# The first sixteen steps of an attention and two-MLP kernel on two tiles of TensorE, with four smaller edits

## The reference, cut to what matters

```
q, k, v: batch 4, heads 8, seq 576, head_dim 64
scores = (q @ k^T) / 8
thresh = max(scores, -1) - tau
scores = where(scores >= thresh, scores, -1e9) - max(scores)
attn   = exp(scores) / (sum(exp(scores)) + 1e-9)
x      = attn @ v                       -> x: 2304 tokens x 512
h  = x @ w_in;   g  = h * sigmoid(1.702 h);      x2  = g @ w_out    (d_ff 2048)
h2 = x2 @ w_in2; g2 = h2 * tanh(softplus(h2));   out = g2 @ w_out2
```

## Time and profile before

| | |
|---|---|
| median of 3 runs | 1164.04 us (1163.72 to 1164.51) |
| the profiled execution's own time | 1164.05 us |
| its span, first to last instruction | 1162.3 us |
| busy PE / PEld / DVE / ACT / POOL | 96 / 89 / 65 / 62 / 25 % |
| mean granted clock of TensorE | 0.995 |
| PE in the slices, tenths | 8978889999999999999999999999999999999998 |

### The profile page before, as it was taken

The page is one execution under the profiler, slowest core; times in us unless marked ns, Lnnn a source line. Parts: engine busy times, 40 slices in busy tenths (PEclk is TensorE's granted clock), DMA queues, the critical chain, the costliest instruction groups (busy, mean ns, idle before and its releaser), DMA issues.

```text
span 1162.3 us, 19359 instructions
## 1 busy us (share of the span) xinstructions
PE 1118.1 (96%) x7472; PEld 1035.4 (89%) x7472; DVE 759.1 (65%) x1359; ACT 724.1 (62%) x995; POOL 295.4 (25%) x502
## 2 busy tenths in 40 slices
PE   8978889999999999999999999999999999999998
PEld 4568889998999999999999999998999989899997
DVE  4678788888888888888888434665433444344343
ACT  3678787767777777777767322467545554554453
POOL 3557674434444433344333000000000000000000
PEclk9989999999999999999999999999999999999999
DMA  2443534232143222233231003520010000000000
GB/s 65 140 131 114 158 86 111 59 94 85 48 111 91 64 82 77 79 105 83 70 103 28 26 19 106 190 76 28 6 49 1 28 28 28 28 28 28 1 28 27
DMA packets 92923, 78.71 MB, mean 68 GB/s; under 512 B 47520, under 2 KB 78752, under 8 KB 92832
## 3 DMA queue, kind: packets, MB, share of 16 engines
q1 hardware_dynamic: 92832, 77.49, 22.9%
HBM read 63.83 MB, written 13.63 MB: 67 GB/s over the span
## 4 chain that ended last, share of the span: by engine, by line
PE 78%; DVE 11%; ACT 7%; issue 3%; POOL 0%; DMA 0%; SPq 0%; ACTq 0%; DVEq 0%
PE ps_s L743 17%; PE ps_r L628 14%; PE ps_r L648 11%; PE ps_r L766 9%; PE ps_t L492 6%; PE ps_t L513 5%; PE ps_t L766 4%; PE ps_s L477 4%; PE ps_t L648 3%; PE ps_r L513 2%; PE ps_s L466 2%; DVE x_pair L585 2%; DVE pt_lo L574 2%; ACT pv_half_sb L544 1%; DVE neg_max L554 1%
## 5 line engine op out<-in xcount | busy, mean ns | idle before, releaser
L628 PE MATMUL ps_r<-x_hi,wi_lo 128*128 128x256 f32 x544 | 158.5, 291 | 2.7 <-DVE x_lo L701 2.7
L810 DVE COPY hidden<-ps_s 128x768 f32<-128x768 f32 x48 | 45.8, 956 | 170.5 <-PE ps_s L743 170.5
L628 PE MATMUL ps_r<-x_lo,wi_hi 128*128 128x256 f32 x544 | 154.2, 284 | 0.0
L628 PE MATMUL ps_r<-x_hi,wi_hi 128*128 128x256 f32 x544 | 154.2, 283 | 0.0
L492 PE MATMUL ps_t<-ident,e_buf 128*128 128x128 f32 x720 | 118.1, 283 | 27.1 <-DVE pt_lo L574 14.5
L839 ACT ACTIVATE m_lo_raw<-m_lo_raw 128x1536 f32<-128x1536 f32 x24 | 35.8, 1491 | 168.8 <-DVE m_lo_raw L817 168.8
L561 DVE SCALAR_TENSOR_TENSOR e_buf<-ps_s,neg_thr,e_buf 128x576 f32<-128x576 f32 x144 | 117.0, 813 | 29.4 <-ACT e_buf L521 22.9
L648 PE MATMUL ps_r<-g_hi,wo_lo 128*128 128x256 f32 x464 | 135.4, 292 | 0.0
L537 ACT CAST pt_hi<-ps_t 128x640 fp32r<-128x640 f32 x128 | 89.0, 695 | 71.8 <-PE ps_t L492 69.6
L743 PE MATMUL ps_s<-x_hi,wi_lo 128*128 128x384 f32 x384 | 129.0, 336 | 2.4 <-DVE x_lo L799 2.4
L492 PEld LDWEIGHTS ps_t<-ident,e_buf 128*128 128x128 f32 x720 | 84.7, 143 | 52.1 <-issue 29.2
(11 more groups left out here) (105 smaller groups left out, 3009.9 us busy)
## 6 DMA issues: line engine op xcount, KB each, us to landing
k_ll_raw<-in_k SPq DMA_DIRECT2D x56, 288.0 KB, 2.9
v_st_raw<-in_v SPq DMA_DIRECT2D x64, 160.0 KB, 2.9
wi_lo_raw<-in_moe_w_in SPq DMA_DIRECT2D x16, 512.0 KB, 3.8
wo_lo_raw<-in_moe_w_out SPq DMA_DIRECT2D x16, 512.0 KB, 4.8
q_raw<-in_q SPq DMA_DIRECT2D x32, 192.0 KB, 2.9
x_scratch<-y_acc SPq DMA_DIRECT2D x9, 512.0 KB, 3.2
x_lo_raw<-x_scratch SPq DMA_DIRECT2D x6, 768.0 KB, 4.7
out_rows<-rows_out SPq DMA_DIRECT2D x18, 256.0 KB, 2.1
```

Source lines behind the costliest of these rows:

```text
L628: mm = pe.matmul(bank[:, part * CH:(part + 1) * CH], wi[w][:, k, f * P:(f + 1) * P], x[:, k, :], start=t == 0, stop=t == 3 * KT - 1)
```

## The change

In the first 16 steps:

- The scores are made in four products of 144 columns rather than two of 288: keys 0 to 287 on rows 0 to 63 of the array, keys 288 to 575 on rows 64 to 127, alternately. So q and k are loaded and scaled on all 128 partitions.
- The product with v alternates between output partitions 0 to 63 (j = 0, 2, 4) and 64 to 127 (j = 1, 3). The two halves are then added as in later steps: `act_pv` copies one, `dve_pv` adds the other. `act_x_first` and its semaphore go. `dve_pv` stands in pass n behind `dve_max(n)`.
- Six float32 products of the identity with itself stand ahead of the first scores, and three more behind each of the passes 0 to 4.

Also: the last `x_hi_first` and `x_lo_first` come a pass sooner (ACT: ahead of `p_hi(16)`; DVE: pass 18), and with them `READY[0]` becomes 18, so that the same 32 halves are spread over the passes 18 to 42. The second half of each key's low part on POOL moves a pass back, behind `pool_row`. One weight's slot moves from 17 to 16, and SP issues weights three rather than four passes ahead.

```diff
-READY = [GROUPS[g][4] + (4 if c == 0 else 8) for c, g in enumerate(CHUNK_GROUP)]
+READY = [GROUPS[g][4] + (3 if c == 0 else 8) for c, g in enumerate(CHUNK_GROUP)]
-        W_SLOT = dict(zip((9, 12, 14, 17, 19, ...), W_ORDER))
+        W_SLOT = dict(zip((9, 12, 14, 16, 19, ...), W_ORDER))
-            q = q_raw[u % 2][0:D, lo:hi]
+            q = q_raw[u % 2][:, lo:hi]
@@ pe_scores
-                for half in range(2):
-                    mm = pe.matmul(scores(n)[:, half, :], q_raw[u0 % 2][0:D, q_cols(h, i)],
-                                   k_raw[u0 % 2][0:D, half * HS:(half + 1) * HS], start=True, stop=True)
+                for part in range(2):
+                    for half in range(2):
+                        rows = slice(half * D, (half + 1) * D)
+                        c = slice(part * HS // 2, (part + 1) * HS // 2)
+                        mm = pe.matmul(scores(n)[:, half, c], q_raw[u0 % 2][rows, q_cols(h, i)],
+                                       k_raw[u0 % 2][rows, half * HS:(half + 1) * HS][:, c], start=True, stop=True)
+        def pe_idle(pe, count):
+            for _ in range(count):
+                pe.matmul(ps_r[:, 1, 384:512], ident[:, :], ident[:, :], start=True, stop=True)
@@ pe_pv, g < H
+                for j in range(NJ):
+                    rows = slice((j % 2) * D, (j % 2 + 1) * D)
+                    mm = pe.matmul(pv_bank(g)[rows, 0:w], v_raw[u % 2][:, j, D:P], pv_moving(g)[0][:, j, :],
+                                   start=j < 2, stop=j >= NJ - 2)
@@ dve_pv
+            if g < H:
+                rows = x_raw[base:base + D, h // 2, 0:w]
@@ PE loop
             pe.wait_ge(s["ident_ready"], 1)
+            pe_idle(pe, 6)
             pe_scores(pe, 0)
...
+                    if n < 5:
+                        pe_idle(pe, 3)
@@ ACT loop
-                    if n >= 2:
+                    if 2 <= n < FRONT + 2:
                         act_p_hi(act, n - 2)
                     if n - 3 in GROUP_AT:
-                        act_x_first(act, GROUP_AT[n - 3])
+                        act_pv(act, GROUP_AT[n - 3])
                     if n in X_HI_FIRST:
                         act_x_hi_first(act, X_HI_FIRST[n])
+                    if n == FRONT + 2:
+                        act_p_hi(act, n - 2)
@@ DVE loop, behind dve_max and the weights' low parts
-                if n - 1 in X_HI_FIRST:
-                    dve_x_lo_first(dve, X_HI_FIRST[n - 1])
+                if n < FRONT + 3 and n - 3 in GROUP_AT:
+                    dve_pv(dve, GROUP_AT[n - 3])
+                for late in (1, 0):
+                    if n - late in X_HI_FIRST and (X_HI_FIRST[n - late] < KT - 1) == (late == 1):
+                        dve_x_lo_first(dve, X_HI_FIRST[n - late])
@@ POOL loop
-                for u in KQ_PREP.get(n, []):
-                    pool_k_lo(pool, u)
+                for half in (1, 0):
+                    for u in KQ_PREP.get(n - half, []):
+                        pool_k_lo(pool, u, half)
@@ SP
-            sp.dma_start(k_raw[u % 2][rows, :], kt[b, h][rows, :]).then_inc(k_in[u % 2], 16)
+            sp.dma_start(k_raw[u % 2], kt[b, h]).then_inc(k_in[u % 2], 16)
-                if n + 4 in W_SLOT:
-                    w_load(sp, 0, W_SLOT[n + 4])
+                if n + 3 in W_SLOT:
+                    w_load(sp, 0, W_SLOT[n + 3])
```

More of the change, by code:

```diff
@@ L239, in thresholded_attention_two_mlps @@
                  "qk_done maxed thr_ready share_ready exped masked eps_ready inverted normed_first normed turned "
-                 "p_hi p_lo pv_done x_first pv_half pv_sum "
+                 "p_hi p_lo pv_done pv_half pv_sum "
                  "x_hi_done x_lo_done up_done tanh_done h_read g_hi_done g_lo_done down_done y_read "
@@ L303, in x1_count @@
             return sum(len(x1_stores(x)) for x in range(g) if x1_place(x) == place)
[L307 to L311, removed]
         def pv_bank(g):
@@ L330, in ring_release @@
                 pe.wait_ge(s["p_lo"], N - FRONT)
-                wait_sums(pe, len(GROUPS))
+                pe.wait_ge(s["pv_sum"], len(GROUPS))
                 return
             if k < 2:
-                wait_sums(pe, H)
+                pe.wait_ge(s["pv_sum"], H)
                 return
@@ L368, in thresholded_attention_two_mlps @@
         W_ORDER = [0, 1, 2, 3, 8, 9, 4, 5, 10, 11, 6, 7, 12, 13, 14, 15]
-        W_SLOT = dict(zip((9, 12, 14, 17, 19, 21, 23, 24, 26, 28, 30, 31, 33, 34, 36, 37), W_ORDER))
+        W_SLOT = dict(zip((9, 12, 14, 16, 19, 21, 23, 24, 26, 28, 30, 31, 33, 34, 36, 37), W_ORDER))
         def w_place(c):
@@ L409, in act_k_hi, with pool_k_lo @@
             act.copy(k_hh[u % 2], k_raw[u % 2]).then_inc(s["k_hi"], 1)
-        def pool_k_lo(pool, u):
+        def pool_k_lo(pool, u, half):
             pool.wait_ge(s["k_hi"], u - H + 1)
-            for half in range(2):
-                c = slice(half * HS, (half + 1) * HS)
-                pool.tensor_tensor(k_ll[u % 2][:, c], k_raw[u % 2][:, c], k_hh[u % 2][:, c].bitcast(F32),
-                                   ALU.subtract).then_inc(s["k_lo"], 1)
+            c = slice(half * HS, (half + 1) * HS)
+            pool.tensor_tensor(k_ll[u % 2][:, c], k_raw[u % 2][:, c], k_hh[u % 2][:, c].bitcast(F32),
+                               ALU.subtract).then_inc(s["k_lo"], 1)
         def act_q_hi(act, u):
@@ L502, in pe_pv @@
                 if g >= 2:
[L503 to L509, removed]
+                    pe.wait_ge(s["pv_sum"], g - 1)
+                for j in range(NJ):
+                    rows = slice((j % 2) * D, (j % 2 + 1) * D)
+                    mm = pe.matmul(pv_bank(g)[rows, 0:w], v_raw[u % 2][:, j, D:P], pv_moving(g)[0][:, j, :],
+                                   start=j < 2, stop=j >= NJ - 2)
+                mm.then_inc(s["pv_done"], 1)
+                return
+            pe.wait_ge(s["p_lo"], last + 1 - FRONT)
+            pe.wait_ge(s["v_lo"], u - H + 1)
+            pe.wait_ge(s["pv_sum"], g)
             parts = pv_moving(g)
@@ L512, in pe_pv @@
                 for part, pt in enumerate(parts):
-                    mm = pe.matmul(pv_bank(g)[out_rows, 0:w], v[:, j, :], pt[:, j, :],
+                    mm = pe.matmul(pv_bank(g)[:, 0:w], v_st[u % 2][:, j, :], pt[:, j, :],
                                    start=j == 0 and part == 0, stop=j == NJ - 1 and part == len(parts) - 1)
@@ L542, in act_pv @@
             act.wait_ge(s["pv_done"], g + 1)
-            wait_sums(act, g)
+            if g >= 1:
+                act.wait_ge(s["pv_sum"], g)
             act.copy(pv_half_sb[base:base + D, 0:w], pv_bank(g)[D:P, 0:w]).then_inc(s["pv_half"], 1)
[L546 to L550, removed]
         def dve_max(dve, n):
@@ L580, in dve_pv @@
             par, grp = x1_place(g)
-            rows = x_pair[base:base + D, grp * 256:grp * 256 + w]
-            dve.wait_ge(s["pv_half"], g - H + 1)
+            dve.wait_ge(s["pv_half"], g + 1)
+            if g < H:
+                rows = x_raw[base:base + D, h // 2, 0:w]
+            else:
+                rows = x_pair[base:base + D, grp * 256:grp * 256 + w]
             if x1_count(g, (par, grp)):
@@ L695, in act_x_hi_first @@
         def act_x_hi_first(act, k):
-            wait_sums(act, 2 * (k + 1))
+            act.wait_ge(s["pv_sum"], 2 * (k + 1))
             act.copy(x_hi[:, k, :], x_raw[:, k, :]).then_inc(s["x_hi_done"], 1)
@@ L919, in _ @@
                 if n - 2 < N:
-                    wait_sums(pe, g + 1)
+                    pe.wait_ge(s["pv_sum"], g + 1)
                     pe_turn(pe, n - 2, range(NJ - 1, NJ))
@@ L1099, in sp_k @@
             b, h, _ = USES[u]
-            rows = slice(0, D if u < H else P)
             if u >= 2:
                 sp.wait_ge(s["qk_done"], LAST[u - 2] + 1)
-            sp.dma_start(k_raw[u % 2][rows, :], kt[b, h][rows, :]).then_inc(k_in[u % 2], 16)
+            sp.dma_start(k_raw[u % 2], kt[b, h]).then_inc(k_in[u % 2], 16)
         def sp_q(sp, u):
             b, h, cols = USES[u]
-            rows = slice(0, D if u < H else P)
             lo, hi = q_span(cols)
@@ L1112, in sp_q @@
                 sp.wait_ge(s["q_lo"], u - H - 1)
-            sp.dma_start(q_raw[u % 2][rows, lo:hi], qt[b, h, rows, lo:hi]).then_inc(q_in[u % 2], 16)
+            sp.dma_start(q_raw[u % 2][:, lo:hi], qt[b, h, :, lo:hi]).then_inc(q_in[u % 2], 16)
         def sp_v(sp, u):
@@ L1145, in _ @@
                         sp_v(sp, u + 2)
-                if n + 4 in W_SLOT:
-                    w_load(sp, 0, W_SLOT[n + 4])
+                if n + 3 in W_SLOT:
+                    w_load(sp, 0, W_SLOT[n + 3])
                 for g in groups_summed(n):
-                    wait_sums(sp, g + 1)
+                    sp.wait_ge(s["pv_sum"], g + 1)
                     par, grp = x1_place(g)
```

## The result

The changed kernel takes 1168.22 us (median of 20 runs, 1165.18 to 1171.31) against 1164.01 (1163.49 to 1164.96): ratio 1.0034, 95 % interval 1.0026 to 1.0041. It is slower by 0.34 %; 1160.0 was forecast. Its runs spread over 6 us, those of before over 1.5.

The account below looks back on a forecast made before the run. The front was taken to go from PE-bound to bound by DVE's wait for the sum. Leads of 1.6 at step 17, 3.8 at step 20 and 0.2 for keys made 4.0: 1164.05 - 4.0 = 1160.0 us, range 1157 to 1162.

Parts of the forecast that it names:

- The loop of DVE and ACT: First 16 steps: mask to mask 2.68 us in odd passes, 4.43 in even ones, where the mask waits for the sum.
- M(7): Start of step 7's threshold mask on DVE, forecast at 30.2 us; M with another number is that step's mask.
- Identity products and doubled loads: Front's start: loads cost 0.6 us, first scores at 4.9, full clock by 5 to 9, step 5's mask 23.1 against 26.80.
- Product with v, 1.45: PE in the front: v product on two output tiles takes 1.45 us rather than 2.30, as six places.
- Scores, 0.80: PE in the front: scores on two row tiles take 0.80 us rather than 1.16, as five places.
- Steady front: Steps 5 to 17: 7.1 us a pair at full clock, step 17's mask at 66.4 against 68.03, lead 1.6.
- rival A: Passes 6 to 16: TensorE's clock falls in pauses the sum opens, 2.5 us per even pass, about 1168 us; chance 0.27.
- Last x a pass sooner: Passes 17 to 20: first MLP half starts sooner, without PE's 2.67 us pause; lead grows from 1.6 to 3.8 us.
- Passes 20 to 43 as before: Stretch averaging 4.50 us a step keeps its pace; keys by halves add 0.2, so the lead is 4.0 at pass 43.
- rival C: Behind pass 20, other waits lose half of the lead at step 17's mask: 1163 us; chance 0.15.
- Behind pass 43 nothing changes: From pass 43 on both kernels issue the same work in the same order, just earlier or later.

## Why the prediction was wrong, step by step

1. **The loop of DVE and ACT, 2.68 a pass, and the sum ahead of the mask:** right. Up to M(7) even passes took 4.34 and 4.45 (forecast 4.43), odd ones 2.65 and 2.68. With the pauses filled the later even ones took 3.99 to 4.45.
2. **Identity products and doubled loads:** right, but for the term of the loads. M(0) 7.78 (7.95), clock up by the second group of identity products (6.2 us), M(5) 22.80 (23.1). Scores(0) came at 4.38, and at 4.48 in the kernel without identity products, against 4.34 before, so the doubled loads cost at most 0.14 where I took 0.6.
3. **Product with v, 1.45:** 1.44 to 1.45.
4. **Scores, 0.80:** 0.69. The rule of my sum, eight instructions in order in five places, was wrong: the places are those of the fuller tile, four for the scores (4 x 0.12 + 0.20 = 0.68) and six for v (three products of two instructions on the one tile). The Trainium skill ("TensorE: Matmul & The Clock Gate", Part 3: Packing small matmuls) had it better; the trace agrees with 0.68, my estimate from that page.
5. **Steady front, 7.1 us a pair up to M(17):** this is the step that failed. The sum took turns, scores and v product at full clock all through; from 29.7 us on every pair of steps ran at half clock for a part of it, each v product in whole or in part. From M(7) to M(17) it took 43.6 us rather than 36.2, since the clock fell with the pauses that item 1 opens; with the pauses filled it took 35.8. I gave that (rival A) 0.27 and 1168 us, its price for an even pass at half clock 2.5 (6.78 - 4.45 = 2.3 measured), and it came out at 1168.2. The mechanism is A's, but that the number is met so closely is in part luck: A had three or four slow passes at the full price, while five were slow in part, by 2.4, 1.5, 1.1, 1.6 and 1.1 against the kernel with the pauses filled, and 1168.2 also holds the loss of item 8, which A did not have. The evidence for the better weight stood in the rows: 1.7 us of pause with little work around it was enough before, and by my own sum PE had 4.45 us of work in 7.1. I set against it one pause of 0.85 between dense products, and a rule of the Trainium skill (same page, "HAM oscillation — how this bites in real kernels") that wants a longer idle gap than any here. The trace contradicts that rule: the clock fell at 29.7 us, in the second of two pauses of 1.16 and 1.63 us with 0.76 of work between them.
6. **Last x a pass sooner, M(17) to M(20) in 13.5:** 13.2, but by two misses that cancel. The first half started 5.2 after M(17) (4.6 forecast), with 0.31 us of idle ahead of it rather than 2.67. M(19) came 9.6 after M(17), where I had 9.0 (8.9 with the clock held), and M(19) to M(20) took 3.6, where I had 4.5.
7. **Passes 20 to 43 as before:** right, 103.8 against 103.5. So rival C's loss did not come there.
8. **Behind pass 43 nothing changes:** wrong by 1.8 us. The lag was 3.3 at M(43) and 5.1 in the spans. I took both kernels to be the same from pass 43 on, but keys by halves goes on to the last step. I priced it at 0.2, for passes 20 to 42 only, where it is 1.5 gained and then 1.4 to 1.9 lost.

What stays open: why the split costs behind pass 44, and what the weight's slot and the later issue of weights do, which were always changed together with the tiles. The traces place the loss between passes 64 and 104, in jumps of 0.4 to 0.8, but the waits of that stretch don't name one cause.

## What to carry to other kernels

Before putting an instruction that waits into an in-order queue, write down what stands behind it; the same sum cost 8 us ahead of the mask and nothing behind the next maximum. A faster product on an engine that is no longer the bound turns into pauses, and on TensorE pauses can cost the clock: compare busy PE in each stretch with stretches in which the clock fell, instead of looking for one long gap, and take the answer as a warning and not as a rule (the last section has why). And follow an edit through all the passes in which it is active, not only those for which it was made.

## What the runs showed of the hardware that I had not expected

- Float32 products on two row tiles start in pairs, the pairs 0.12 us apart for 144 columns at 2.4 GHz, though each product is two instructions on its tile; the two halves of 576 keys took 0.69 rather than 1.16 us.
- Turns and scores on one tile did not raise the clock in 12 us back to back; with the scores on two tiles it rose at some 17.6 us, in spite of pauses and without any identity products. That is one trace.
- Identity products raised the clock in one execution and not in another. In the kernel before with identity products alone, the first two steps' scores behind them took 2.21 us (full clock); in the kernel with all but the tiles, behind the same twelve instructions, 4.17 (half). The times of these two one-tile kernels scatter over 6 to 7 us, those of the seven two-tile kernels whose clock was not driven down by the sum over 0.7 to 1.7.
- The length of one pause does not settle what the clock does. In the kernel before, a pause of 1.68 us (59.0 to 60.7) was followed by a v product at half clock (4.06 us); in the kernel with all but the tiles a pause of 1.93 us at the same place (60.1 to 62.0) was followed by one at full clock (2.37).
